# Gated linear attention ahead of two expert layers: y computed token by token, the router's logits as extra columns of v, and the state kept head by head

## The reference

```python
f = 1.0 / (1.0 + np.exp(-f_logit))
for t in range(S):
    state = f[:, :, t, :, None] * state + np.einsum('bhd,bhe->bhde', k[:, :, t], v[:, :, t])
    y[:, :, t] = np.einsum('bhd,bhde->bhe', q[:, :, t], state)
...
logits = x @ w_gate + modality_bias[modality_id]
e_idx = np.argmax(logits, axis=1)
```

## Time and profile before

| what | value |
|---|---|
| median of 3 runs | 860.41 us (859.09 to 861.08) |
| the profiled execution | 857.94 us, span of its instructions 856.2 us |
| PE busy over the span | 821.0 us (96%) |
| DVE, ACT, POOL busy | 471.3, 385.9, 127.4 us |
| attention | from the start to about 152 us of the span |
| the two expert layers | the rest |

### The profile page before, as it was taken

The page is one execution under the profiler, slowest core; times in us unless marked ns, Lnnn a source line. Parts: engine busy times, 40 slices in busy tenths (PEclk is TensorE's granted clock), DMA queues, the critical chain, the costliest instruction groups (busy, mean ns, idle before and its releaser), DMA issues.

```text
span 856.2 us, 15107 instructions
## 1 busy us (share of the span) xinstructions
PE 821.0 (96%) x5300; PEld 750.8 (88%) x5300; DVE 471.3 (55%) x782; ACT 385.9 (45%) x742; POOL 127.4 (15%) x143
## 2 busy tenths in 40 slices
PE   6899997789999999989999999999999999999997
PEld 6788886779999999989888888888888888888887
DVE  8999997778767666643544343343334334333332
ACT  5888886455665555553323312331231223123112
POOL 3012113248444000010000200100020010001001
PEclk9999999999999999999999999999999999999999
DMA  9877756698987787732000100200020000000000
GB/s 190 175 157 181 169 133 240 224 364 251 306 257 244 263 319 268 243 98 71 22 1 14 61 1 1 73 0 0 0 73 0 0 37 0 0 0 37 0 0 37
DMA packets 44086, 96.54 MB, mean 113 GB/s; under 512 B 9168, under 2 KB 25040, under 8 KB 43920
## 3 DMA queue, kind: packets, MB, share of 16 engines
q1 hardware_dynamic: 39952, 85.81, 34.2%
q0 software_dynamic: 3840, 9.47, 3.1%
q10 hardware_dynamic: 256, 0.79, 0.3%
HBM read 76.75 MB, written 19.29 MB: 112 GB/s over the span
## 4 chain that ended last, share of the span: by engine, by line
PE 78%; issue 2%; DVE 1%; DMA 1%; SPq 0%; POOL 0%; ACT 0%; DVEq 0%; ACTq 0%
PE h_ps L1771 16%; PE h_ps L1773 16%; PE h_ps L1772 16%; PE ym_ps L1771 7%; PE ym_ps L1773 7%; PE ym_ps L1772 7%; PE xTm_ps L1772 3%; PE xTm_ps L1771 3%; PE xTm_ps L1773 3%; PE xT_ps L1788 1%; PE xTm_ps L1779 1%; DMA w_in<-in_w 1%; POOL out L1434 0%; ACT w_hi L1452 0%; SPq L1292 0%
## 5 line engine op out<-in xcount | busy, mean ns | idle before, releaser
L1746 DVE TENSOR_TENSOR gs<-h_ps,sig 128x512 f32<-128x512 f32 x72 | 49.8, 691 | 176.2 <-ACT sig L1546 176.2
L1546 ACT ACTIVATE sig<-h_ps 128x512 f32<-128x512 f32 x72 | 43.1, 598 | 159.5 <-PE h_ps L1773 159.5
L1557 ACT CAST h_hi<-hid 128x512 fp32r<-128x512 f32 x72 | 44.6, 620 | 149.6 <-DVE hid L1749 149.6
L1771 PE MATMUL h_ps<-x_hi,w_hi 128*128 128x256 f32 x312 | 89.3, 286 | 7.2 <-DVEq L1673 3.8
L1773 PE MATMUL h_ps<-x_lo,w_hi 128*128 128x256 f32 x312 | 89.2, 286 | 0.0
L1772 PE MATMUL h_ps<-x_hi,w_lo 128*128 128x256 f32 x312 | 89.0, 285 | 0.0
L1771 PE MATMUL h_ps<-w_hi,wg_hi 128*128 128x512 f32 x216 | 85.5, 396 | 0.0
L1773 PE MATMUL h_ps<-w_lo,wg_hi 128*128 128x512 f32 x216 | 84.6, 392 | 0.0
L1773 PE MATMUL h_ps<-w_lo,wv_hi 128*128 128x512 f32 x216 | 84.2, 390 | 0.0
L1771 PE MATMUL h_ps<-w_hi,wv_hi 128*128 128x512 f32 x216 | 84.0, 389 | 0.0
L1772 PE MATMUL h_ps<-w_hi,wv_lo 128*128 128x512 f32 x216 | 84.0, 389 | 0.0
(11 more groups left out here) (231 smaller groups left out, 1831.1 us busy)
## 6 DMA issues: line engine op xcount, KB each, us to landing
w_raw<-in_w SPq DMA_DIRECT2D x52, 384.0 KB, 5.1
w_in<-in_w SPq DMA_DIRECT2D x52, 384.0 KB, 5.4
qkf_in<-in_qkf SPq DMA_DIRECT2D x43, 288.0 KB, 5.0
y_sorted<-x_group SPq DMA_DIRECT2D x13, 384.0 KB, 3.4
v_in<-in_v SPq DMA_DIRECT2D x24, 192.0 KB, 4.6
x_regions<-zero_row SPq DMA_DIRECT2D x12, 384.0 KB, 3.4
x_group<-x_regions SPq DMA_DIRECT2D x12, 384.0 KB, 3.9
g_in<-in_wg SPq DMA_DIRECT2D x3, 768.0 KB, 7.7
```

The lines of the kernel that those rows point to most:

```text
L1546: nc.scalar.activation(sig[:], g_ps, ACT.Sigmoid).then_inc(sig_done, 1)
L1557: nc.scalar.copy(h2_hi[:, fb % HELD], hid[:]).then_inc(h2_hi_done, 1)
L1746: nc.vector.tensor_tensor(gs[:], g_ps, sig[:], ALU.mult).then_inc(gs_done, 1)
L1771: nc.tensor.matmul(out, hi, rhs_hi, start=first, stop=False)
```

## The change

The product that made yT swaps its operands: `scores` is now the stationary operand and v the moving one, so that y comes out with tokens on partitions. The columns that move are 48 of v and 8 of v times the head's part of the gate weights, which makes the router's partial logits come out beside y (`VG` = 56). Those 8 columns per head are made by a new product per pair (`gate_pair` moving, v transposed, `vT_in`, stationary) and copied by ACT behind v in `v_in`. v arrives padded to 56 columns per head and a second time as `vT`. The copy of yT and the turning product go. The state and its growth are kept per head, 48 rows by 56 columns, instead of as a pair's 112 by 112 block. The x copy and the logits reduction move from three to two steps behind, the program has two steps fewer at the end, `choose` and `place` stand two and one steps earlier, the group's scatters are written in one loop, and the preparation for the first expert tile is spread differently over the last steps. The start loses the zeroing of `grown` and `yT_ps` on DVE and gets the gate loads ahead of the first v.

```diff
-        v_in = sb("v_in", [P, B, DM])
+        v_in = sb("v_in", [P, B, H, VG])
+        vT_in = sb("vT_in", [2 * D, B, PR, P])
+        gate_pair = sb("gate_pair", [2 * D, PR, 2 * E])
...
-        state = sb("state", [P, B, PR, P])
-        grown = sb("grown", [P, B, PR, P])
+        state = sb("state", [P, B, PR, VG])
+        grown = sb("grown", [P, B, PR, VG])
         fade = sb("fade", [P, B, PR])
-        yT = sb("yT", [P, 2, PR, P])
-        turn_gate = sb("turn_gate", [P, PR, XG])
...
-        ks_ps = ps("ks_ps", [P, PR, P])
+        turn_ps = ps("turn_ps", [P, 512])
         sc_ps = ps("sc_ps", [P, 2, 2, PR, P])
-        yT_ps = ps("yT_ps", [P, PR, P])
-        ds_ps = ps("ds_ps", [P, 512])
-        x_ps = ps("x_ps", [P, 512])
-
-        def x_pairs(n):
-            bank = yT_ps[:].rearrange("p j t -> p (j t)") if n == NT - 1 else x_ps
-            return bank[:, 0:PR * XG].rearrange("p (j r) -> p j r", j=PR)
-
-        rt_ps = x_ps[:, PR * XG:PR * XG + 2 * E].rearrange("p (i e) -> p i e", i=2)
-        flag_ps = ds_ps[:, DM:DM + 1]
+        ds_bank = ps("ds_ps", [P, 512])
+        x_ps = ps("x_ps", [P, 2, 512])
+
+        ks_ps = turn_ps[:, 0:PR * ROWS].rearrange("p (j d) -> p j d", j=PR)
+        vg_ps = turn_ps[:, PR * ROWS:PR * ROWS + H * E]
+        ds_ps = ds_bank[:, 0:PR * VG].rearrange("p (j d) -> p j d", j=PR)
+        x_heads = x_ps[:, :, 0:PR * VG].rearrange("p r (j d) -> p r j d", j=PR)
+        rt_ps = x_ps[:, 0, PR * VG:PR * VG + 2 * E].rearrange("p (i e) -> p i e", i=2)
+        flag_ps = ds_bank[:, DM:DM + 1]
...
             def load_v(c, b, n):
 
                 wait_past(sp, y_done, n - 3)
-                sp.dma_start(v_in[:, b], v[n]).then_inc(v_landed[b], 16)
+                sp.dma_start(vT_in[:, b].rearrange("p j t -> p (j t)"), vT[n]).then_inc(v_landed[b], 16)
+                sp.dma_start(v_in[:, b].rearrange("p h d -> p (h d)"), v[n]).then_inc(v_landed[b], 16)
...
+            sp.wait_ge(consts, GATES)
+            for par in range(2):
+                sp.dma_start(gate_pair[par * D:(par + 1) * D, :, par * E:(par + 1) * E], w_gate[par]).then_inc(wg_in, 16)
+            load_v(0, 0, 0)
             second_load(sp, 0)
-            load_v(0, 0, 0)
             sp.wait_ge(pads_set[3], 2)
             load(0, 3)
...
-                if (t := tile(c, b, 1)) and t[2] < GROWN:
+                if t := tile(c, b, 1):
                     _, s, n = t
                     act.wait_ge(k_turned, n + 1)
-                    wait_past(act, ds_done, n - 3)
-                    nc.scalar.copy(ks[:, s, :, 0:ROWS], ks_ps[:, :, 0:ROWS]).then_inc(ks_done, 1)
+                    if n < GROWN:
+                        wait_past(act, ds_done, n - 3)
+                        nc.scalar.copy(ks[:, s, :, 0:ROWS], ks_ps)
+                    nc.scalar.copy(v_in[:, s, :, D:VG], vg_ps.rearrange("p (h e) -> p h e", h=H)).then_inc(ks_done, 1)
...
-                        last = nc.scalar.activation(state[:, s, j], grown[:, s, j], ACT.Copy,
-                                                    scale=fade[:, s, j:j + 1])
+                        last = nc.scalar.activation(state[0:ROWS, s, j], grown[0:ROWS, s, j], ACT.Copy,
+                                                    scale=fade[0:ROWS, s, j:j + 1])
...
+                if t := tile(c, b, 2):
+                    cc, s, n = t
+                    act.wait_ge(y_done, n + 1)
+                    if cc > 1:
+
+                        act.wait_ge(scattered[s], (cc - 1) * 16)
+                    nc.scalar.copy(rt.x[:, cc % 2, s, :].rearrange("p (j r d) -> p r j d", j=PR, r=2),
+                                   x_heads[:, :, :, 0:D]).then_inc(x_copied, 1)
...
-                    for r, d in ((0, 0), (PAD, D)):
-                        ds = ds_ps[:, 0:DM].rearrange("p (j e) -> p j e", j=PR)
-                        last = nc.vector.tensor_tensor(grown[r:r + D, s, :, r:r + D], ds[r:r + D, :, d:d + D],
-                                                       state[r:r + D, s, :, r:r + D], ALU.add)
-                    last.then_inc(grown_done, 1)
-                if at(c, CH) and b == 1:
...
-                    nc.vector.tensor_reduce(rt.logits[:, n, :], x_pairs(n)[:, :, 2 * D:XG].rearrange("p j e -> p e j"),
-                                            AX.X, ALU.add).then_inc(x_kept, 1)
+                    nc.vector.tensor_reduce(rt.logits[:, n, :], x_heads[:, :, :, D:VG].rearrange("p r j e -> p e r j"),
+                                            AX.XY, ALU.add).then_inc(x_kept, 1)
...
-                if b == B - 2 and not (at(c, 0) or at(c, CH)):
+                if b == 1 and not (at(c, 0) or at(c, CH)):
 
                     dve.wait_ge(x_kept, c * B)
                     rt.choose(nc, dve, c - 1, marks, (c - 1) * Routing.PLACED)
-                if b == 0 and not (at(c, 0) or at(c, 1)):
-                    dve.wait_ge(counted, c - 1)
-                    rt.place(nc, dve, c - 2, half, rt_ps[:, 0], rt_ps[:, 1], marks, (c - 2) * Routing.PLACED)
-                    if c == CH - 1:
+                if b == B - 1 and not at(c, 0):
+                    dve.wait_ge(counted, c)
+                    rt.place(nc, dve, c - 1, (c - 1) % 2, rt_ps[:, 0], rt_ps[:, 1], marks, (c - 1) * Routing.PLACED)
+                    if c == CH - 2:
...
-                if isinstance(n, int) and n == 0:
-                    pe.wait_ge(v_landed[0], 16)
-                    pe.wait_ge(ks_done, 1)
                 wait_past(pe, grown_done, n)
                 for j in range(PR):
-                    mm = nc.tensor.matmul(ds_ps[0:ROWS, 2 * D * j:2 * D * (j + 1)], ks[:, s, j, 0:ROWS],
-                                          v_in[:, s, 2 * D * j:2 * D * (j + 1)], start=True, stop=True)
+                    for par in range(2):
+                        r, end = (0, PAD) if par == 0 else (PAD, ROWS)
+                        mm = nc.tensor.matmul(ds_ps[r:end, j], ks[:, s, j, r:end], v_in[:, s, 2 * j + par],
+                                              start=True, stop=True)
                 mm.then_inc(ds_done, 1)
 
-            def read(c, b, t, acc):
-                cc, s, n = t
+            def read(cc, s, n):
+                if n < GROWN:
+                    growth(s, n)
+
+                wait_past(pe, x_kept, n)
+                if cc > 0:
+                    wait_past(pe, state_done, n - 3)
+                    for j in range(PR):
+                        for par in range(2):
+                            r = PAD * par
+                            nc.tensor.matmul(x_heads[:, par, j], qT[r:r + D, s, j], state[r:r + D, s, j], start=(j == 0), stop=False,
+                                             skip_group_check=True)
                 pe.wait_ge(masked, n + 1)
-                if at(c, 0):
-                    pe.wait_ge(consts, CONSTS)
-                pe.wait_ge(v_landed[s], (cc + 1) * 16)
-                if n < GROWN and n > 0:
-                    growth(s, n)
-
-                wait_past(pe, state_done, n - 3)
-                if not at(cc, 0):
-                    for j in range(PR):
-                        nc.tensor.matmul(acc[0:ROWS, j], state[0:ROWS, s, j, 0:ROWS], qT[0:ROWS, s, j], start=(j == 0), stop=False,
-                                         skip_group_check=True)
-                if at(cc, 0):
-                    pe.wait_ge(yT_zero, 1)
                 for j in range(PR):
                     for par in range(2):
-                        h, r = 2 * j + par, PAD * par
-                        mm = nc.tensor.matmul(acc[r:r + D, j], v_in[:, s, D * h:D * (h + 1)],
-                                              scores[:, s % 2, par, j], start=at(cc, 0), stop=(at(cc, 0) or j == PR - 1),
-                                              skip_group_check=True)
+                        mm = nc.tensor.matmul(x_heads[:, par, j], scores[:, s % 2, par, j], v_in[:, s, 2 * j + par],
+                                              start=(cc == 0 and j == 0), stop=True, skip_group_check=True)
                 mm.then_inc(y_done, 1)
 
-            def step(c, b, half):
+            def step(c, b):
                 if t := tile(c, b, 1):
-                    _, s, n = t
+                    cc, s, n = t
+                    if n == 0:
+                        pe.wait_ge(wg_in, 32)
+                    pe.wait_ge(v_landed[s], (cc + 1) * 32)
+                    wait_past(pe, ks_done, n)
+                    for j in range(PR):
+                        mm = nc.tensor.matmul(vg_ps[:, 2 * E * j:2 * E * (j + 1)], vT_in[:, s, j], gate_pair[:, j], start=True, stop=True)
+                    if n < GROWN:
+                        pe.wait_ge(scaled, n + 1)
+                        for j in range(PR):
+                            mm = nc.tensor.transpose(ks_ps[:, j], kT[0:ROWS, s, j], ident[0:ROWS, 0:ROWS])
+                    mm.then_inc(k_turned, 1)
...
-                if t := tile(c, b, 3):
-                    _, s, n = t
-                    if at(c, 0):
```

(28 more changed lines are left out.)

138 lines of the change are left out of this document (52 added, 86 removed).

## The result

The changed kernel takes **983.27 us** (median of 4 runs, 979.94 to 985.69), the kernel before 859.75 in the same comparison (4 runs): a ratio of 1.143 [1.140, 1.147]. The forecast was 868, with a range of 859 to 876: the right side, and far too little. The next stage, whose start stood at 152.22, now starts at 275.92, 123.7 us later, and the profiled span grew by 122.0 (856.2 to 978.2). So everything was lost inside attention; the expert layers only moved.

A forecast was written before the change was run, and what follows sets the result against it. PE was taken to bound attention, its step growing from 5.38 to 6.08 us with tile 3 ending as before. The next stage came 7.9 us later: 857.94 + 7.9 = 865.9, and 2.5 more for the median, 868.3; range 859 to 876.

The forecast's parts named there:

- The step that failed: Attention, 60 to 90 us: granted clock read as 1.00 (2.4 GHz) and carried over to the changed step.
- A pass costs 98 to 123 ns by its stationary side, not by what moves: PE in attention: an untiled pass with 128 stationary columns doesn't get below about 110 ns, however few columns move.
- The additive rival: PE's y and gate products: load and moving columns add up, 0.98 us a step, 888 us; chance 4%.
- the rule that it cites: Trainium skill page: a weight load overlaps a matmul only in another row group; y about 0.7 us more a step, unused.
- Growth: PE's growth group, 16 passes: loads follow one another, 0.79 us a step as before; low 0.45, high 1.01.
- rival "cheap": Growth and state read run their array parts together: step 5.62 us, 860.6 us in all, no change; chance 12%.
- Tile 18 at 131.8, tile 21 at 147.7, `place` at 149.7: Dates in us late in attention when these tiles and `place` end, from steps of 6.08 us and the routing counts.
- the four counts: Routing counts between tiles 4 and 18: 3.6 us together beyond the plain steps, 0.9 each.
- The start: Attention up to tile 3: DVE's dropped zeroing (1.76 us) pays for tile 2's later load (some 2); y ends at 37.0.
- Next stage at 160.1: Start of the stage after attention: the old 10.4 us behind `place` at 149.7, so 7.9 us later than before.
- The other side: PE's y passes are not held up by their load: step near 5.1 us, 4.5 us faster, about 856; chance 8%.
- DMA as the bound: Attention's loads don't pass 190 GB/s: a tile takes 6.4 us, the start 2 to 3 more, 875 us; chance 15%.

The follow-up runs named there:

- experiment 9: The changed kernel with four unread filler products of 128 moving columns added in each step ahead of the state read: 939.50 and 963.93 us.
- experiment 7: The changed kernel with y and state read widened to 112 columns, the opening waits filled and the last v loads ahead of the first expert's weights: 876.15 us.
- experiment 1: The changed kernel with the opening waits filled (32 opening products for 22, 18 more before tile 1's gate product): 944.45 and 965.09 us.
- 4: The kernel before with 1 opening product in place of 22: 862.95 us, ratio 1.002.
- experiment 5: The kernel before with only growth, state and state read made head by head: 852.73 us, ratio 0.991.
- experiment 2: The changed kernel with each y product moving 112 columns in place of 56, the opening not filled: 883.51 us, ratio 1.026.
- 13: The changed kernel with four unread filler products a step that move only 8 columns each: 1025.3 us.
- 11: The changed kernel with growth, state and read in pairs of heads as before, so the y part alone: 901.46 us, ratio 1.048.
- 6: The changed kernel with the state read moving 112 columns in place of 56, y left at 56: 983.72 us, ratio 1.141.
- 8: The changed kernel without the gate product and its copy, so the router's logits are not computed: 943.14 us.
- experiment 3: The changed kernel with each y product moving 112 columns and the opening waits filled: 882.27 us, ratio 1.023.
- 12: The changed kernel with eight unread filler products of 128 moving columns in each step: 950.35 us.
- 14: The changed kernel with growth, state and read in pairs of heads as before, and the opening filled: 884.66 us, ratio 1.026.

## Why the prediction was wrong, step by step

- **The step that failed** is the one that was made in passing: that attention runs "at the full clock (1.00, the 2.4 GHz level)". It was read from the kernel before and carried over as if it belonged to the chip. It belongs to the stream of products, and the change replaces that stream. No rival of mine let it move. One step takes 10.98 us at 0.50 and 5.94 at 1.00 (experiment 9), 1.85 times. Beside experiment 7, which kept the clock to 152.0, the changed kernel's next stage starts 108.0 us later (275.92 for 167.96), and its time is 107 us longer. That is the clock's share of the 123.7 us; the other 15.7 are lost at the full clock too, twice the 7.9 of the forecast. (Experiment 7 is another kernel in the widths and in the place of the last v loads, so the split is an estimate.)
- **What lowers the clock.** Shown: a fall can follow a wait, but a wait isn't needed for it (experiment 1: the fall comes in the midst of a busy stretch), and it doesn't keep the clock down where the stream is another (4, 5 and 2 are back at 1.00 by 20.4, 21.1 and 29.0 us). It isn't the number of passes (5 has the changed step's 76 and runs at 1.00; more of them with 8 columns do nothing, 13), nor the sum of the columns that move (11 moves the same 5,312 and comes back), nor columns through partly filled passes (6), nor the gate group alone (8). Wider products through the full array bring it back, be they y's (2, 3) or unread ones, the latter in part (9, 12). The change took passes that moved 104 (L770), 96 (L704) and 128 columns (y and the read) out of the step and put 16 and 56 in. Experiments 5, 11 and 14 say that neither half of the change alone keeps the clock down as the two together do: the state part alone runs at 1.00 from 21.1 us on, and the y part alone reaches it at 65.5 us, or at 32.9 with the opening filled. Open: why the filler makes it waver where wide y holds it, though the filler moves rather more columns through the full array in a step (8 passes of 128 against 16 x 56 added).
- **A pass costs 98 to 123 ns by its stationary side, not by what moves**: right. y took 1.83 us where 1.77 was forecast, with 112 columns 1.87; gate 0.87 for 0.89, read 1.03 for 1.0, turn 0.51, scores 1.10. The additive rival falls: y's 56 further columns in experiment 2 cost 2 to 3 ns a pass. The 0.7 us that the prediction gives y by the rule that it cites comes without its working; by its own 0.96 ns a column it would be 0.86 for y. Nothing rests on it.
- **Growth**: forecast 0.79, measured 0.60, so tiled passes of 64 and 48 columns do overlap (rival "cheap", partly true). Step: 5.94 against 6.08 forecast.
- **Tile 18 at 131.8, tile 21 at 147.7, `place` at 149.7**: experiment 7 has 132.1, 147.9 and 149.9. That looks exact, and it is luck: two errors cancel. Tile 3 ended its y at 40.2 there, not at 37.0, 3.2 us late; the 14 tiles from 4 to 18 then took 85.9 us, not 88.7, of which 1.4 are the steps (5.98 for 6.08) and 1.4 the four counts (0.55 each for 0.9). The 0.9 was read as PE's work, but 0.45 of it was idle time of PE in front of L118.
- **The start** was the second error. The prediction set DVE's zeroing against a later load of tile 2 and left PE's wait for v out of the sum, though it had it among the signs of being wrong. The wait is there, 2.27 and 3.89 us in front of the gate product. The filling doesn't help there: tile 1's gate product starts at 20.07 without it and at 20.06 with it (experiment 7).
- **Next stage at 160.1**: the third error, 7.9 us even in experiment 7 (167.96). The prediction added the old 10.4 us behind `place`, taken as set by the scatters, and called the work on PE and the splits behind it "just inside". They are outside: PE waits 2.82 us for `x_ahead`, whose load SP issued at 144.13 behind eight loads of weights, the clock falls at 152.0, PE's last y ends at 163.3 and not at 156.1, and `w_lo` comes at 164.74. With the changed kernel's own order of loads it is later still: in experiment 3, where the last v loads stand behind the weights, the next stage starts at 174.70. So a changed kernel that kept its clock through the steady steps would have taken some 876 to 882 us and not 868, an estimate from the times of experiments 7 and 3.
- **The other side** (y's passes cheap) falls: they took 114 ns each. **DMA as the bound** of the step falls: the share is 0.42 in the changed kernel, and experiment 2 has no idle time on PE at 0.81 and a step of 5.93.
- **DVE** did what was said: growth's instruction 382 ns (0.38), the wait in front of the reduction hidden, and at the full clock it is busy 48.76 of 60 us (experiment 2), the forecast 80%. Two of its groups and ACT's new copy between 96 and 118 us, which answer to the earlier trace rows:

```profile
L597 DVE TENSOR_TENSOR grown<-ds_ps,state 112x224 f32<-112x224 f32 x2 | 0.8, 382 | 0.0
L601 DVE TENSOR_REDUCE logits<-x_ps 128x8 f32<-128x64 f32 x2 | 0.5, 225 | 10.6 <-ACT x_group L537 10.6
L519 ACT COPY v_in<-turn_ps 128x64 f32<-128x64 f32 x2 | 0.4, 216 | 0.0
```

So the change has three parts by price: the state head by head is worth 0.9% (experiment 5); y token by token costs 0.6 us of PE a step at the full clock (5.98 against 5.38), 2.6% with the opening filled (14, the lost clock at its end included); and the two together lose the clock through all of attention, some 12% more (983.27 against experiment 7's 876.15).

## What to carry to other kernels

Read the granted clock as a property of the instruction stream, not of the stage: when a change swaps wide-moving full-array products for narrow ones, give a halved clock its own rival, priced at nearly twice PE's step; here a 100% busy PE was the symptom, not the reassurance. When PE's unchanged groups (here the scores) have doubled in duration, stop looking for waits. When a forecast date comes true, check the dates before it: errors may have cancelled. And try a mixed change's halves apart: one was a gain of 8 us, hidden under a loss of 123.

## What the hardware did that I had not expected

- With PE busy 60.00 of 60 us in each window from 60 to 240 us, the granted clock stood at 0.50, in one piece of 266 us; in experiment 1 it fell from 1.00 to 0.50 in the midst of such a busy stretch.
- Adding work made the kernel faster: 16 x 56 more columns a step, 983 to 884 us; four unread products a step, 983 to 940 and 964.
- A halved clock does not double every group: scores took 2.01 for 1.10 and y 3.45 for 1.83, but growth 1.03 for 0.60, the step 10.98 for 5.94, 1.85 times.
- An untiled pass with 128 stationary columns took 114 ns with 56 moving and 117 with 112; with 128, as in the filler, 136 (124 in the doubled filler).
